# Routed network of a three-stage kernel: transposes of rows and of the first layer's output as pairs of half-height ones

## The reference

```python
# 1: gated linear attention, state (48 x 48) per head, 4 batches x 8 heads, 768 steps
state = alpha[t] * state + outer(k[t], v[t]);  y[t] = q[t] @ state
x = y.transpose(0, 2, 1, 3).reshape(3072, 384)
# 2: routed network, 8 experts, d=384, hidden 1024; the best expert of each row
xn, en = x / (norm(x) + 1e-6), expert_emb / (norm(expert_emb) + 1e-6)
probs = softmax(xn @ en.T / tau);  e = argmax;  gate = probs[e]
out[rows of e] = gate * (relu(x[rows of e] @ w1[e]) @ w2[e])
# 3: dense network, hidden 2048
h = out @ w_in;  g = where(h > 0, h, exp(min(h, 0)) - 1);  result = g @ w_out
```

## Time and profile before

| | us |
|---|---|
| three runs, median (range) | 916.39 (916.35 to 917.9) |
| the profiled execution's own time | 914.58 |
| its span in the trace | 913.0 |
| PE busy | 883.1 (97% of the span) |
| DVE, ACT, POOL busy | 434.6, 321.9, 272.8 |
| mean granted TensorE clock | 0.992 |

### The profile page before, as it was taken

One profiled execution on the slowest core, in us unless ns is written; L12 is line 12 of the kernel. 1 busy time (PEld: TensorE's weight loads), 2 busy tenths in 40 slices (PEclk: granted clock), 3 DMA queues, 4 the chain that ended last, 5 costly groups with the idle time before them and its releaser, 6 DMA issues. The chain is left out here.

```text
span 913.0 us, 16295 instructions
## 1 busy us (share of the span) xinstructions
PE 883.1 (97%) x5725; PEld 777.3 (85%) x5725; DVE 434.6 (48%) x826; ACT 321.9 (35%) x708; POOL 272.8 (30%) x279
## 2 busy tenths in 40 slices
PE   7999999889999999999998999999999999999995
PEld 5777888678998998989987989989999999999894
DVE  7777878862222232232224545445445445445442
ACT  4466656532322222232222323323223223223221
POOL 3113344546537644645807301001001001001001
PEclk9999999989999999999999999999999999999998
DMA  9986875948877888756807201002002002000000
GB/s 149 149 130 116 161 130 106 299 184 276 251 242 237 265 277 272 247 166 182 226 27 209 69 1 62 9 1 70 1 1 70 1 0 70 1 1 35 1 1 34
DMA packets 140975, 107.92 MB, mean 118 GB/s; under 512 B 103354, under 2 KB 129074, under 8 KB 140898
## 3 DMA queue, kind: packets, MB, share of 16 engines
q0 software_dynamic: 25696, 66.09, 22.8%
q1 hardware_dynamic: 115202, 40.79, 21.1%
HBM read 89.51 MB, written 17.35 MB: 117 GB/s over the span
## 5 line engine op out<-in xcount | busy, mean ns | idle before, releaser
L1395 POOL DMA_INDIRECT out<-of,idi x24 | 23.6, 983 | 370.2 <-DVE of L1481 305.5
L1215 PE MATMUL bank<-WX,hdTh 128*128 (+1 forms) x496 | 129.0, 341 | 3.6 <-DVE hdTl L1268 2.4
L1439 PE MATMUL bank<-xT_h,wi_h 128*128 128x512 f32 x288 | 114.1, 396 | 0.0
L1439 PE MATMUL bank<-xT_l,wi_h 128*128 128x512 f32 x288 | 113.6, 394 | 0.0
L1439 PE MATMUL bank<-xT_h,wi_l 128*128 128x512 f32 x288 | 113.3, 394 | 0.0
L1499 ACT ACTIVATE ee<-bank 128x512 f32<-128x512 f32 x96 | 57.4, 598 | 147.4 <-PE bank L1439 144.5
L1521 DVE TENSOR_SCALAR em<-ee 128x512 f32<-128x512 f32 x96 | 44.4, 462 | 136.5 <-ACT ee L1499 134.3
L1201 PE MATMUL bank<-WX,xdTh 128*128 (+1 forms) x372 | 100.9, 407 | 1.3 <-issue 1.2
L1502 ACT ACTIVATE g_h<-gg 128x512 fp32r<-128x512 f32 x96 | 60.6, 631 | 115.4 <-DVE gg L1526 112.2
L1139 POOL TENSOR_TENSOR WX<-raw_w,WX 128x3072 fp32r<-128x3072 f32 x14 | 95.6, 6832 | 17.3 <-DMA WX<-moe_w 12.3
L1530 DVE TENSOR_TENSOR g_l<-gg,g_h 128x512 fp32r<-128x512 f32 x96 | 69.2, 721 | 60.2 <-ACT g_h L1502 59.3
(11 more groups left out here) (212 smaller groups left out, 1443.5 us busy)
## 6 DMA issues: line engine op xcount, KB each, us to landing
WX<-moe_w POOLq DMA_DIRECT2D x14, 1536.0 KB, 10.0
raw_w<-moe_w POOLq DMA_DIRECT2D x14, 1536.0 KB, 8.0
xd<-sorted_x SPq DMA_DIRECT2D x31, 193.0 KB, 5.1
sorted_y<-yd SPq DMA_DIRECT2D x31, 192.5 KB, 4.3
xg<-sorted_y SPq DMA_DIRECT2D x6, 770.0 KB, 4.4
nat_a<-alpha SPq DMA_DIRECT2D x32, 144.0 KB, 3.3
nat_k<-k SPq DMA_DIRECT2D x32, 144.0 KB, 3.4
nat_q<-q SPq DMA_DIRECT2D x32, 144.0 KB
```

The lines of the kernel that those rows point to most:

```text
L1215: last = pe.matmul(y_out(t)[:, 0:DM], hdT[a][:, k * P:(k + 1) * P], WX[:, bass.ds(off + (b * WE + KD * F + k * DM), DM)], start=(k == 0 an ...
L1439: last = pe.matmul(bank[4 + i % 2][:, :], a[:, k, w], b[:, k, :], start=(k == 0 and m == 0), stop=(k == KD - 1 and m == 2))
```

## The change

The change concerns tiles from 2 on.

1. Each 128 x 128 transpose of `XT` and `HT` becomes two: rows 0 to 63 and rows 64 to 127 of the data are transposed apart, with 64 rows of the array each (array rows 0 to 63 and 64 to 127, `tile_position`), 128 stationary columns and 64 moving columns (a 64 x 64 piece of the identity). The first half goes to one bank and the second to the neighbouring bank, at the same columns. So `XT` has 6 matmuls and `HT0` and `HT1` have 8 each.
2. The PSUM tensors are declared so that banks 1 and 2 are one tensor, `pair_h`, and banks 6 and 7 another, `pair_x`. `XT` writes `pair_x`.
3. `Xe` and `He` read both banks of a pair through a pattern of runs of 64 columns and write in the order that the matmuls want. `He0` takes the left half of both banks and `He1` the right half. So `He0` and `He1` now both wait for `HT1`, ACT's `He1` waits for DVE's `He0`, and `HT0` and `HT1` of the next tile wait for DVE's `He1`.
4. PE's list for tile t becomes `HT0(t), HT1(t), XT(t+2), M10(t+1), M11(t+1), M2(t)`: `XT` stands ahead of `M10` instead of behind `M11`.
5. The last tile's `M2` writes bank 3 instead of bank 1.

```diff
@@ -240,7 +240,12 @@
         for x in (a_at, d_at, e_at, r_at):
             assert x[0] <= nc.sbuf_usable_end
 
-        bank = [ctx.enter_context(nc.psum_tensor(f"bank{i}", [P, COLS], F32)) for i in range(8)]
+        bank = [ctx.enter_context(nc.psum_tensor("bank0", [P, COLS], F32))]
+        pair_h = ctx.enter_context(nc.psum_tensor("pair_h", [P, 2, COLS], F32))
+        bank += [pair_h[:, h, :] for h in range(2)]
+        bank += [ctx.enter_context(nc.psum_tensor(f"bank{i}", [P, COLS], F32)) for i in range(3, 6)]
+        pair_x = ctx.enter_context(nc.psum_tensor("pair_x", [P, 2, COLS], F32))
+        bank += [pair_x[:, h, :] for h in range(2)]
 
         s_const = sem("s_const")
         s_c0 = sem("s_c0")
@@ -1160,11 +1165,26 @@
                         hold(po, peD.sems["M2" if x else "M11"], end, pool_waits)
                         upper_load(po, k + 1, e, x)
 
+        HP = P // 2
+
+        def by_halves(pair, lo, hi):
+
+            return pair[:, :, lo // 2:hi // 2].rearrange("p h (m t) -> p m h t", t=HP)
+
+        def in_halves(t):
+            return t.rearrange("p (m h t) -> p m h t", h=2, t=HP)
+
+        def xt_all(t):
+            return bank[7 if t else 0][:, 0:DM] if t < EARLY else by_halves(pair_x, 0, DM)
+
+        def ht_half(i, t):
+            return bank[1 + i][:, :] if t < EARLY else by_halves(pair_h, i * F // 2, (i + 1) * F // 2)
+
+        def as_read(x, t):
+            return x if t < EARLY else in_halves(x)
+
         def y_out(t):
-            return bank[5 if t < TILES - 1 else 1]
-
-        def xt_bank(t):
-            return bank[7 if t == 1 else 0]
+            return bank[5 if t < TILES - 1 else 3]
 
         def pe_d(pe):
             def position(t):
@@ -1181,7 +1201,12 @@
                     if t == 1:
                         acA.wait(pe, "yT1", PAIRS - 1)
                     for k in range(KD):
-                        last = pe.transpose(xt_bank(t)[:, k * P:(k + 1) * P], x[:, k * P:(k + 1) * P], ident[:, :])
+                        if t < EARLY:
+                            last = pe.transpose(xt_all(t)[:, k * P:(k + 1) * P], x[:, k * P:(k + 1) * P], ident[:, :])
+                            continue
+                        for h in range(2):
+                            rows = slice(HP * h, HP * (h + 1))
+                            last = pe.transpose(pair_x[:, h, k * HP:(k + 1) * HP], x[rows, k * P:(k + 1) * P], ident[rows, rows], tile_position=(HP * h, 0))
                     return last
                 if name[0:2] == "M1":
                     i = int(name[2])
@@ -1218,10 +1243,15 @@
                     return last
                 i = int(name[2])
                 acD.wait(pe, f"Re{i}", t)
-                veD.wait(pe, f"He{i}", t - 1)
+                veD.wait(pe, f"He{i}" if t <= EARLY - 1 else "He1", t - 1)
                 for m in range(KF // 2):
                     k = KF // 2 * i + m
-                    last = pe.transpose(bank[1 + i][:, m * P:(m + 1) * P], hd[:, k * P:(k + 1) * P], ident[:, :])
+                    if t < EARLY:
+                        last = pe.transpose(bank[1 + i][:, m * P:(m + 1) * P], hd[:, k * P:(k + 1) * P], ident[:, :])
+                        continue
+                    for h in range(2):
+                        rows = slice(HP * h, HP * (h + 1))
+                        last = pe.transpose(pair_h[:, h, k * HP:(k + 1) * HP], hd[rows, k * P:(k + 1) * P], ident[rows, rows], tile_position=(HP * h, 0))
                 return last
 
             def do(*steps):
@@ -1238,13 +1268,15 @@
                 if name == "Xe":
                     peD.wait(ac, "XT", t)
                     peD.wait(ac, "M11", t - 2)
-                    return ac.activation(xdT[t % 2][0][:, :], xt_bank(t)[:, 0:DM], ACT.Copy)
+                    return ac.activation(as_read(xdT[t % 2][0][:, :], t), xt_all(t), ACT.Copy)
                 i = int(name[2])
                 cols = slice(i * COLS, (i + 1) * COLS)
                 if name[0:2] == "He":
-                    peD.wait(ac, f"HT{i}", t)
+                    peD.wait(ac, f"HT{i}" if t < EARLY else "HT1", t)
                     peD.wait(ac, "M2", t - 1)
-                    return ac.activation(hdT[0][:, cols], bank[1 + i][:, :], ACT.Copy)
+                    if i and t >= EARLY:
+                        veD.wait(ac, "He0", t)
+                    return ac.activation(as_read(hdT[0][:, cols], t), ht_half(i, t), ACT.Copy)
                 peD.wait(ac, f"M1{i}", t)
                 peD.wait(ac, f"HT{i}", t - 1)
                 return ac.activation(hd[:, cols], bank[3 + i][:, :], ACT.Relu)
@@ -1260,12 +1292,12 @@
             def step(name, t):
                 if name == "Xe":
                     acD.wait(ve, "Xe", t)
-                    return ve.tensor_tensor(xdT[t % 2][1][:, :], xt_bank(t)[:, 0:DM], xdT[t % 2][0][:, :].bitcast(F32), ALU.subtract)
+                    return ve.tensor_tensor(as_read(xdT[t % 2][1][:, :], t), xt_all(t), as_read(xdT[t % 2][0][:, :].bitcast(F32), t), ALU.subtract)
                 if name[0:2] == "He":
                     i = int(name[2])
                     cols = slice(i * COLS, (i + 1) * COLS)
                     acD.wait(ve, f"He{i}", t)
-                    return ve.tensor_tensor(hdT[1][:, cols], bank[1 + i][:, :], hdT[0][:, cols].bitcast(F32), ALU.subtract)
+                    return ve.tensor_tensor(as_read(hdT[1][:, cols], t), ht_half(i, t), as_read(hdT[0][:, cols].bitcast(F32), t), ALU.subtract)
                 peD.wait(ve, "M2", t)
                 if t >= 2:
                     ve.wait_ge(s_yd[t % 2], t // 2 * 16)
@@ -1596,7 +1628,7 @@
                     e(-1, 0)
                     d(("M2", t))
                 elif t < TILES - 2:
-                    d(("M10", t + 1), ("M11", t + 1), ("XT", t + 2), ("M2", t))
+                    d(("XT", t + 2), ("M10", t + 1), ("M11", t + 1), ("M2", t))
             rounds_e(e, {"H0": lambda: d(("M2", TILES - 1))})
 
 
```

## The result

The changed kernel takes **920.51 us** (median of 6 runs, 919.97 to 921.76), beside 916.18 us (6 runs, 914.4 to 917.9) for the kernel before on the same chip. The ratio is 1.0052, with a 95% interval of 1.0039 to 1.0065: slower, by 0.4 to 0.65%. 922.3 was forecast; the measured ratio on the 916.39 us that the forecast started from gives 921.2.

The account below looks back on a forecast made before the run. PE's time was taken as the bound. 26 rounds losing 0.22 us each, plus 0.2, less 0.2, made 5.7 to 6 us lost, so 922.3 us from 916.39; range 920.3 to 924.5, reaching to B 918.5 to 927.5.

Parts of the forecast that it names:

- Pair of halves, 0.06 us; the halves beside each other: HT and XT: two half-height transposes overlap, and a pair takes 0.06 us, bounded by loading 128 stationary columns.
- rivals B and C: B: a pair costs 0.11 us, 926.8 us, chance 0.12. C: halves don't overlap at all, 956 us, chance 0.02.
- Array alone: Without the sequencer's delay, M10 starts 1.07 us after M2's last matmul starts, its second at 1.41; 0.22 us gained a round.
- Load of `kth` at 0.46: M10's load waits behind 22 short matmuls; with 1.05 us latency M10 starts at 1.51; 0.22 us lost a round.
- The place in the queue: PE's queue has 17 places, each freed as a matmul starts, so M10's load goes out when the 5th half starts.
- Rival A: The queue takes 22 or more short matmuls, M10's load stays hidden, 0.22 us gained a round: 910.7 us, chance 0.09.
- HT of tiles 29 and 30: These two tiles' HT, with 16 matmuls and no XT, gain about 0.05 us each.
- Idle time: M10 and M11's line idles for "issue" some 26 times, about 0.35 us each, 9 us in sum.
- He joined: ACT's and DVE's copies and subtractions run one behind the other but finish before M2 wants them; worth nothing.
- XT earlier: XT(t+2) ahead of M10 causes no wait: DVE's Xe(t+1) ends 2.6 us before M2's last matmul starts.
- loads of M11 and M2: The later loads of kth, at about 2.2 and 3.9 us, stay hidden behind M10 and M11.
- Clock: The granted clock stays at 2.4 GHz; nothing is charged for the new gaps of 0.44 us.

Follow-up runs that it names:

- x9: x1 without the upper halves of HT, eight half-height matmuls instead of 16: 911.69 us in one run beside 914.72, round 9.387 us.
- x1: The changed kernel with one load of kth for M10 and M11, issued ahead of HT0: 913.56 us, ratio 0.994 to the kernel before.
- x4: The kernel before with XT, in whole transposes, moved ahead of M10 and nothing else: 917.91 us, ratio 0.9991.
- x5: The kernel before with the early, single load of kth for M10 and M11 ahead of HT0: 918.43 us, ratio 0.9996.
- x15: x1 with the load of kth behind the 15th of HT's 16 halves: 920.57 us in one run beside 914.72, round 9.753 us.
- x2: The changed kernel with one load of kth for M10 and M11 between HT1 and XT, behind 16 halves: 923.43 us, ratio 1.0059.
- x3: The changed kernel with XT back behind M11, 16 halves ahead of the load: 935.03 us, ratio 1.0173 to the kernel before.
- x6: x1 with all lower halves ahead of all upper ones in each of HT0, HT1 and XT: 914.41 us, ratio 0.9952.
- x14: x1 with the load of kth behind the 14th of HT's 16 halves: 913.53 us in one run beside 918.1, round 9.387 us.

## Why the prediction was right

The direction was right, and so was the mechanism that makes the loss: M10 waits for a load of `kth` that goes out too late behind the short matmuls. The size was nearly right. What holds the load up was not what the prediction took it to be, and there the number was luck. By its own steps:

- **Pair of halves, 0.06 us; the halves beside each other.** Right: 0.0625 (x9's lower halves, and HT to XT in x1: 0.55 us for eight pairs, with the first load in it). This closes rivals B and C. The Trainium skill's rule in "TensorE: Matmul & The Clock Gate", section on LDWEIGHTS, columns over 1.2 ns, would have made 0.11 of each pair; the trace decides against it for these transposes.
- **Array alone: M10 at 1.07, second matmul at 1.41, 0.22 gained a round.** Nearly right: x1 has 1.10 and 1.44. With the 0.327 of XT (x4) in place of 0.35, 0.15 late less 0.33 is 0.18, and 0.18 was measured.
- **Load of `kth` at 0.46, latency 1.05, M10 at 1.51, second matmul at 1.85: 0.22 lost a round.** The mechanism is shown by x1 and x5, the size was too large. The load came at 0.42 (0.27 + 0.15), the latency was 1.02 in most rounds, M10 started at 1.43 and its second matmul at 1.77. That is 0.48 late, less 0.33 for XT is 0.15; 0.163 was measured, 26 of which are 4.2 us (4.5 by the means of the rounds, 9.741 and 9.569) where 5.7 to 6 stood in the sum. The mis-sized terms are the load's moment and the latency, 0.03 to 0.04 us each.
- **The place in the queue.** The prediction had the 22nd half handed over as the 5th starts. The load is found when four have started, so 18 lie ahead. This step was wrong, and its number right by luck. x15 shows that the rule "17 matmuls lie ahead" itself fails at the change of array: the 15th half waits for HT to start, and from there it is the sequencer's own pace, not a place in the queue, that puts the load 0.146 us behind HT. The 5th half starts 0.174 behind HT, so behind 22 the two rules come out at nearly the same moment, and the forecast didn't suffer. With 16 halves ahead of the load (x2, x3) they don't: the rule of 17 gives 0.42 us ahead of HT, and no loss. Rival A would have needed the queue to take short matmuls more freely. Ahead of HT's start it takes them less freely. The depth of 64 that the Trainium skill gives in "TensorE: Matmul & The Clock Gate" is not seen in any run here.
- **HT of tiles 29 and 30 gain 0.05 each.** Wrong for tile 29, and by this same rule: 16 halves stand ahead of the load, it goes out with HT's start (479.98), and M10 waits. The load:

```profile
L1191 PEldq TENSOR_LOAD <-kth x1: 302/302/302, 480.0 to 480.0; - x1
```

and PE in order of time there:

```profile
479.71 0.34 PE L1240 MATMUL bank<-WX,hdTl 128*128 x1
479.98 0.71 PE L1254 MATMUL pair_h<-ident,hd 64*128 64x64 f32 x16
481.01 0.73 PE L1226 MATMUL bank<-WX,xdTh 128*128 x2 [0.33 <-issue]
```

The second matmul of M10 came 0.35 later than before (1.64 against 1.29). Tile 30 gained 0.03.
- **Idle time: 26 times, 9 us in sum.** 28 times and 8.5 us.
- **He joined, XT earlier, loads of M11 and M2: nothing.** Right: no wait of PE in a regular round but the one for issue, and ACT and DVE have 0.60 and 0.69 us an instruction as before (1.09 for two that overlap, 1.29 for two). XT(3) was 0.19 dearer (0.66 us from M10's last matmul to M11's first, where it was 0.48, and 0.015 behind it), as the 0.2 of the prediction had it. The first round gained 0.18, not 0.1.
- **Clock.** Unchanged, 0.991 against 0.992 over the span.

The forecast's level was 1.1 us above 916.39 x 1.0052 = 921.2. It had added 5.9 us, and the rows of the two executions have 4.9 in their place: the 26 regular rounds lost 4.5, not 5.7 to 6, and tiles 29 and 30 together lost 0.3 where 0.1 was to be gained. The two misses partly cancel.

## What to carry to other kernels

When instructions are made shorter and more numerous, look for a register load behind them on the same sequencer: count how many must be handed over before it, and ask whether those already in the queue still run longer than the load's latency (here 1.02 us from load to first matmul). If they don't, place the load ahead of the run of short instructions; here that was worth 1.1% of the kernel, more than the 0.6% that the halves and the early load gain together over the kernel before, and it costs nothing where the load was hidden (x5). A change that loses may hold a gain under its new wait.

## What the runs showed of the hardware

- Halves of the array run on their own. Two matmuls of XT started before HT's last, which stands ahead of them in the program and left the upper half free (x9), and all lower halves ahead of all upper ones cost only 0.05 us a round (x6).
- With whole and half-height matmuls mixed in the queue, 14 halves were taken behind M2's last matmuls by the same count of 17 as before; the 15th only as the array had gone over to halves, 0.6 us later than the count gives (x14 against x15), be it a half or a whole one (x9). Once it had, 18 lay ahead in the changed kernel. The cause was not found.
- The change of the array delays the first half-height matmul by 0.09 us (HT starts 0.27 after M2's last matmul, 0.176 before), and M10's first one behind the last pair by about as much again.
- A register load costs no time on the array where it is early, 3.1 us ahead (x5), 1.2 (x4) or 0.77 (x14). It was paid for in all kernels where it came as HT started or later.
